# Attention, an MLP in Strassen form and a gated MLP on one core: GpSimd splits the second weight and Moe2's weights, and products take their data in pairs

## The chip, the cores and the metric

The kernel runs on one core of a Trainium2 chip. The metric is the device time of one execution in microseconds (us); the kernel before takes 808.46 us, the median of 3 runs (808.29 to 809.04). A core has a matrix engine (TensorE, PE in the rows; PEld is its weight load), a vector engine (VectorE, DVE), an activation engine (ScalarE, ACT), a general engine (GpSimd, POOL), and a queue engine (SyncE, SP) that here issues every DMA. Each engine executes its own list of instructions in order and waits for the others on semaphores.

## What is computed

```python
# stage 1: attention, B=4, H=8, S=576, D=64, causal window of 128, ALiBi bias
scores = scale * q @ k.T ; scores = where(mask, scores + bias, -1e9)
attn = exp(scores - max) ; attn = attn / (sum(attn) + 1e-9) ; out = attn @ v
x = out as (4, 576, 512)
# stage 2: Moe
h = (x.T @ U @ V).T ; u = x + h                 # rank 32
x = u + maximum(u @ w_ch1, 0) @ w_ch2           # 512 -> 2048 -> 512
# stage 3: Moe2
h = maximum(x @ w_in, 0) ; u, v = halves of h   # 512 -> 1024
v_n = (v - mean(v)) / sqrt(var(v) + 1e-6)
v_s = einsum('ts,bsd->btd', w_spatial, v_n) + b_spatial
out = (u * v_s) @ w_out
```

## The kernel before, in words

All matrix products from stage 2 on are done on fp32 numbers that are split in two: a high part (a copy into a reduced format) and a low part (the number minus its high part). A product is three matmuls: high by high, low weight by high data, high weight by low data. So each operand, data and weight, needs two passes before it can be used, a copy and a subtraction.

**The phases.** First comes attention, 16 pairs of heads, in `step`, a pipeline over three pairs. Then "up" (`u @ w_ch1`) in 24 units (G = 3 groups of 768 tokens, 8 units each), then "down" (`relu(...) @ w_ch2`) in 3 groups, then Moe2 for 4 batches. Up and down each use seven half-sized products in place of eight (Winograd's form of Strassen). The products are numbered m = 1 to 7. For them sums of blocks are needed, on the data side (`x_sum`, `r_sum`) and on the weight side: four sums S1 to S4 beside the blocks A11, A12, A22.

**Up.** A unit s is seven products of 6 matmuls, in the order (s,1), (s-1,4), (s-1,3), (s,2), (s,6), (s,5), (s,7). Between them ScalarE copies partial sums out of PSUM (`keep_p`, L934, into `sums_u`), VectorE adds and writes the four result blocks of a unit to a stage of two slots (`c11`, `c12`, `c22`), ScalarE the fourth (`c21`), and SP stores the stage to DRAM (`store_r(s)`, L421). A slot is free only when the store of two units before has landed (`room`, which waits for `r_out`): `c11(s)` waits for it, `c22(s)` stands behind `c11(s)` on VectorE, and product (s,3) waits for `c22(s)`. At the change of a group (units 8 and 16) VectorE also makes the sums and low parts of the new group's data (`x_sum`, `lo_xs`, L1271).

**The second weight.** In units 9 to 14, 17 and 18 (`W2_UNIT`) one eighth of `w_ch2` is loaded into `w1raw`. VectorE makes its four sums, ScalarE the high parts into `w2_top` (`w2_shi_of` L925, `w2_hi_of` L918, L919), VectorE the low parts, and SP stores all to DRAM (`store_w2`, `w_scr`). `w2_top` is one buffer: ScalarE waits for `w2_out` (the stores of the eighth before) at the head of `w2_shi_of`, and the `keep_p(s, 6)` of the unit stands behind it on ScalarE.

**Down.** At the end of up, the results of the first group come back from DRAM (`load_raw`, blocks a, b, d into `tok`, c into `raw_c`), the weight parts into `w2q[m]` (2 MB each), and `u` into `u_in`. For each of 8 parts kk of a product, ScalarE writes the high part (`hi_r`) and VectorE the low part (`lo_r`) of 384 columns into a ring of 5 (`rk`), and TensorE does 6 matmuls. The sums `r_sum` go by halves of 4 parts, 1536 columns; the first (`r_sum(0, 3, 0)`, L1405) stands right behind the fourth `lo_r` of the first product and reads `raw_c`. `add_res` (L1429) needs `u_in`.

**Moe2.** Its 17 weight pieces are loaded late (in the last group of down) into `w1raw`, four slots. ScalarE copies the high part (`hi_wc`, L984), GpSimd subtracts (`lo_wc`, L710). Beside this GpSimd has only the low parts in attention and, late, some of `v`. In each batch: `half_v`, `half_u`, `spatial`, `output`.

The order on each engine is that of the code below: nothing is scheduled by a planner.

Of the kernel before, what the change touches and what calls it, by code (L numbers as in the profile page):

```python
# [42 lines left out]
RING = 5  # L43
# [20 lines left out]
def rows(t):  # L64
    return P if t < TILES - 1 else TAIL
# [23 lines left out]
DN_AT = {x: (n + 1) * UNITS for n, x in enumerate(DN)}  # L89
ENTRY = {x: n * UNITS for n, x in enumerate(DN)}  # L90
ENTRIES = [(g, m, kk) for g, m in DN for kk in range(UNITS)]


W2_UNIT = {9: 0, 10: 1, 11: 2, 12: 3, 13: 4, 14: 5, 17: 6, 18: 7}
W2_AT = {kk: s for s, kk in W2_UNIT.items()}
# [3 lines left out]
def program(nc, qk, v_n, mu, mv, w1, w2, w_in, w_sp, b_sp, w_out, out_t, u_scr, r_scr, w2_scr, x2_scr):  # L99
    ctx = ExitStack()  # L100
    with ctx:
# [40 lines left out]
        pu.close()  # L142
        pl = ExitStack()
        pl.enter_context(nc.sbuf_tensor("gap1", [P, 15744], F32))
        late = sb(pl, "late", [P, 2, 4, HT], F32)
# [4 lines left out]
        w2q = {4: sb(pd, "w2q4", [P, 2, UNITS, QP], F32R)}  # L150
        raw_c = sb(pd, "raw_c", [P, UNITS, HT], F32)
        u_in = sb(pd, "u_in", [P, 2, 2, HT], F32)
        sums_d = sb(pd, "sums_d", [P, 3, 2, HT], F32)
        pd.enter_context(nc.sbuf_tensor("gap2", [P, 896], F32))
        rk = sb(pd, "rk", [P, RING, 2, HT], F32R)
        for m in (3, 1, 2, 6, 5, 7):
            w2q[m] = sb(pd, f"w2q{m}", [P, 2, UNITS, QP], F32R)
# [9 lines left out]
        wsh = sb(pc, "wsh", [P, TILES, S], F32R)  # L167
        wsl = sb(pc, "wsl", [P, TILES, S], F32R)
# [48 lines left out]
        w2q_in = {m: sem(f"w2q_in{m}") for m in range(1, 8)}  # L217
# [5 lines left out]
        w2_out = sem("w2_out")  # L223
# [11 lines left out]
        pool_passed = sem("pool_passed")  # L235
# [66 lines left out]
        vl_pad = sem("vl_pad")  # L302
# [40 lines left out]
        def r_stage(s, n=slice(0, 4)):  # L343

            if s >= LATE:
                return late[:, s % 2, n, :]
            return tok[:, n, s % 2 * HT:(s % 2 + 1) * HT]
# [10 lines left out]
        def w2_sums(kk):  # L358
# [4 lines left out]
                  tok[:, 0:4, 2 * HT:2 * HT + QP]]  # L363

# [4 lines left out]
        def _(sp):  # L369
# [31 lines left out]
            for r in range(4):  # L401
                sp.dma_start(mvraw[r * RANK:(r + 1) * RANK, :], mv).then_inc(mix_in, 16)
            load_qk(0, 2)
            load_w1(0)
            load_qk(0, 3)
            load_v(0, 2)
            load_w1(1)
# [15 lines left out]
            def load_w2(kk):  # L423
# [4 lines left out]
                else:  # L428
                    sp.wait_ge(w2_out, 6 * 16 * (kk - 1))
# [4 lines left out]
            def store_w2(kk):  # L434
                sp.wait_ge(w2_slow, kk + 1)
                sp.wait_ge(w2_low, 2 * (kk + 1))
                ra, rb = w2_of(kk)
                low = [ra[:, 0:QP], rb.rearrange("p (q c) -> p q c", c=QP), w2_sums(kk)]
                for h, parts in ((0, w2_top), (1, low)):
                    sp.dma_start(w2_scr[A11, :, h, kk, :], parts[0]).then_inc(w2_out, 16)  # L440
                    sp.dma_start(w2_scr[A12:A22 + 1, :, h, kk, :].rearrange("q p c -> p q c"),
                                 parts[1]).then_inc(w2_out, 16)
                    sp.dma_start(w2_scr[S1:S4 + 1, :, h, kk, :].rearrange("q p c -> p q c"),
                                 parts[2]).then_inc(w2_out, 16)

            def load_w2q(m):
                sp.dma_start(w2q[m][:].bitcast(F32), w2_scr[WEIGHT[m]]).then_inc(w2q_in[m], 16)
# [6 lines left out]
            def next_raw(g, n, h):  # L454

                last = {"a": (g - 1, 5), "b": (g - 1, 7), "c": (g - 1, 3), "d": (g - 1, 4)}[n]
                sp.wait_ge(rk_lo, ENTRY[last] + 4 * h + 4)
# [27 lines left out]
            def load_wc(m):  # L485
                slot = m % 4
# [1573 lines left out]
```

## Time and profile before

| | |
|---|---|
| median of 3 runs | 808.46 us |
| the profiled execution: time, span | 811.25 us, 809.5 us |
| busy PE, DVE, ACT, POOL | 91%, 61%, 47%, 12% |
| mean granted TensorE clock | 0.966 |
| moved by DMA | 119.20 MB, mean 147 GB/s |

The profile's picture of the span in 40 slices (20.2 us each; digits are tenths busy; PEclk is the granted TensorE clock in tenths of full speed):

```profile
PE   8999999889998788895589999979879999999998
DVE  6877787877675566321586896795827436416422
ACT  5977787635443343322235455536535233342322
POOL 1611136700000000000000000121331010000100
PEclk9999999999999899898779999999999999999999
DMA  6433242345368876599855625623460010000101
```

Slices 1 to 7 are attention, 8 to 18 up, 19 to 29 down, 30 to 40 Moe2. A matmul's end is modelled, so a PE that is 9 in ten may still have small holes, but where the digit is under 9, TensorE stood still.

### The profile page before, as it was taken

Reading aid. Unit: us, or ns where it says so; the run is one execution under the profiler, and the core shown is the slowest. Engines: PE = TensorE matmul, PEld = TensorE weight load, DVE = VectorE, ACT = ScalarE, POOL = GpSimd, SP = SyncE. Lnnn points to the kernel's source line nnn. Section 1 sums busy time; section 2 is a strip of 40 time slices with the busy share of each in tenths; the row PEclk is TensorE's granted clock in tenths of the full one; section 3 lists DMA queues with packets and bytes.
Section 4 is the critical chain, followed back from the end, with each engine's and each line's share of the span. In section 5 each row is a group of like instructions: output and inputs, shape, how many; then the busy total and the mean of one; then the engine's idle time right before and its main releaser. Section 6 shows DMA issues by size and latency. Waiting matters only on the chain.

```text
span 809.5 us, 13413 instructions
## 1 busy us (share of the span) xinstructions
PE 739.8 (91%) x4688; PEld 678.3 (84%) x4688; DVE 491.4 (61%) x1149; ACT 377.8 (47%) x889; POOL 97.5 (12%) x77
## 2 busy tenths in 40 slices
PE   8999999889998788895589999979879999999998
PEld 5777777789997778894589989969869899899998
DVE  6877787877675566321586896795827436416422
ACT  5977787635443343322235455536535233342322
POOL 1611136700000000000000000121331010000100
PEclk9999999999999899898779999999999999999999
DMA  6433242345368876599855625623460010000101
GB/s 205 124 110 103 88 152 73 130 156 183 120 234 279 284 241 206 192 384 421 313 183 191 195 77 197 246 65 121 131 247 1 1 60 1 25 34 0 58 0 59
DMA packets 74547, 119.20 MB, mean 147 GB/s; under 512 B 4992, under 2 KB 56704, under 8 KB 73600
## 3 DMA queue, kind: packets, MB, share of 16 engines
q1 hardware_dynamic: 74496, 118.55, 42.7%
q8 instruction: 29, 0.48, 0.2%
q14 instruction: 22, 0.18, 0.1%
HBM read 70.82 MB, written 47.71 MB: 146 GB/s over the span
## 4 chain that ended last, share of the span: by engine, by line
PE 70%; DVE 10%; DMA 10%; issue 4%; SPq 3%; ACT 3%; POOL 0%; DVEq 0%; ACTq 0%
PE bank L1840 4%; PE bank L1841 4%; PE bank L1842 4%; PE bank L1682 4%; PE wide L1697 3%; PE bank L1878 3%; PE bank L1880 3%; PE bank L1879 3%; PE bank L1989 2%; PE bank L1664 2%; DMA w_scr<-tok 2%; PE bank L1991 2%; PE bank L1990 2%; PE bank L1807 2%; PE bank L1805 2%
## 5 line engine op out<-in xcount | busy, mean ns | idle before, releaser
L1840 PE MATMUL bank<-xs,w1s 128*128 128x384 f32 x336 | 118.7, 353 | 20.0 <-ACT sums_u L934 15.8
L953 ACT ACTIVATE rk<-tok 128x384 fp32r<-128x384 f32 x144 | 73.6, 525 | 97.5 <-PE wide L1880 48.7
L1841 PE MATMUL bank<-xs,w1s 128*128 128x384 f32 x336 | 116.7, 347 | 0.0
L1842 PE MATMUL bank<-xs,w1s 128*128 128x384 f32 x336 | 116.5, 347 | 0.0
L1878 PE MATMUL bank<-rk,w2q 128*128 128x384 f32 x208 | 73.1, 351 | 32.0 <-DVE rk L1393 28.3
L1840 PEld LDWEIGHTS bank<-xs,w1s 128*128 128x128 f32 x336 | 66.4, 198 | 24.4 <-ACT sums_u L934 18.3
L796 ACT ACTIVATE sc<-sc,mn 128x256 f32<-128x256 f32 (+1 forms) x144 | 67.0, 468 | 20.7 <-DVE mn L1167 20.6
L934 ACT ACTIVATE sums_u<-bank 128x384 f32<-128x384 f32 x72 | 35.2, 489 | 83.0 <-PE bank L1842 80.0
L1878 PEld LDWEIGHTS bank<-rk,w2q 128*128 128x128 f32 x208 | 40.2, 193 | 37.5 <-DVE rk L1393 30.5
L1880 PE MATMUL bank<-rk,w2q 128*128 128x384 f32 x208 | 71.1, 342 | 0.0
L1879 PE MATMUL bank<-rk,w2q 128*128 128x384 f32 x208 | 71.1, 342 | 0.0
L1841 PEld LDWEIGHTS bank<-xs,w1s 128*128 128x128 f32 x336 | 66.6, 198 | 0.0
L1842 PEld LDWEIGHTS bank<-xs,w1s 128*128 128x128 f32 x336 | 66.4, 198 | 0.0
L1396 DVE TENSOR_TENSOR rk<-tok,rk 128x384 fp32r<-128x384 f32 x96 | 51.0, 564 | 23.0 <-ACT rk L953 23.0
L710 POOL TENSOR_TENSOR wvl<-w1raw,wvh 128x512 fp32r<-128x512 f32 x4 | 7.5, 1896 | 362.8 <-ACT wvh L984 362.8
L1167 DVE CUSTOM_DVE_ANT_0 sc<-bank,bias 128x256 f32<-128x256 f32 (+1 forms) x128 | 42.3, 384 | 5.4 <-PE bank L1644 3.5
L1176 DVE COPY pt<-bank 128x512 f32<-128x512 f32 x48 | 31.4, 682 | 20.8 <-PE bank L1682 20.8
L1878 PE MATMUL wide<-rk,w2q 128*128 128x384 f32 x128 | 43.3, 338 | 0.6 <-DVE rk L1396 0.5
L1880 PE MATMUL wide<-rk,w2q 128*128 128x384 f32 x128 | 43.0, 336 | 0.0
L1879 PE MATMUL wide<-rk,w2q 128*128 128x384 f32 x128 | 43.0, 336 | 0.0
L1879 PEld LDWEIGHTS bank<-rk,w2q 128*128 128x128 f32 x208 | 40.3, 194 | 0.0
L1880 PEld LDWEIGHTS bank<-rk,w2q 128*128 128x128 f32 x208 | 40.2, 193 | 0.0
(222 smaller groups left out, 1830.7 us busy)
## 6 DMA issues: line engine op xcount, KB each, us to landing
r_scr<-tok SPq DMA_DIRECT2D x19, 768.0 KB, 4.1
w2q<-w_scr SPq DMA_DIRECT2D x7, 2048.0 KB, 14.5
tok<-r_scr SPq DMA_DIRECT2D x18, 768.0 KB, 5.8
qkraw<-qk SPq DMA_DIRECT2D x32, 288.0 KB, 3.0
w1raw<-w SPq DMA_DIRECT2D x32, 256.0 KB, 3.7
w_scr<-tok SPq DMA_DIRECT2D x12, 512.0 KB, 3.5
u_scr<-tok SPq DMA_DIRECT2D x6, 768.0 KB, 4.6
raw_c<-r_scr SPq DMA_DIRECT2D x6, 768.0 KB, 4.6
```

What stands on the lines that cost most here:

```text
L796: act.activation(w, w, ACT.Exp, bias=mn[:, s, n:n + 1], scale=-1.0, accum_out=sm[:, i, c:c + 1]).then_inc(exp_done, 1)
L934: act.activation(sums_u[:, i, :], a_ps[s % 2][:, 0:HT], ACT.Copy).then_inc(kept, 1)
L953: act.activation(rk[:, n % RING, 0], raw[RAW_OF[m]][:, kk, :], ACT.Relu if m <= 3 else ACT.Copy).then_inc(rk_hi, 1)
L1167: dve.tensor_tensor_reduce(out=out, in0=src, in1=add, scale=-SCALE, scalar=3e38, op0=ALU.add, op1=ALU.min, accum_out=mn[:, s, n:n + 1]).th ...
L1396: dve.tensor_tensor(lo, x, hi, ALU.subtract).then_inc(rk_lo, 1)
L1682: last = pe.transpose(pt_ps[f % 2][:, j * P:(j + 1) * P], sc[:, i % 2, n, w * P:(w + 1) * P], ident[:, :])
L1840: pe.matmul(o, wh, ah, start=(k == 0 and m in FRESH), stop=False, skip_group_check=True)
L1841: pe.matmul(o, wl, ah, start=False, stop=False, skip_group_check=True)
L1842: last = pe.matmul(o, wh, al, start=False, stop=(k == 1), skip_group_check=True)
L1878: pe.matmul(o, wh, rh, start=(kk == 0 and m in FRESH), stop=False, skip_group_check=True)
L1879: pe.matmul(o, wl, rh, start=False, stop=False, skip_group_check=True)
L1880: last = pe.matmul(o, wh, rl, start=False, stop=(kk == UNITS - 1), skip_group_check=True)
```

## The change

- The second weight is no longer split on ScalarE and VectorE but wholly on GpSimd, in `split_w2`: 4 sums, 4 copies, 4 subtractions. It runs through the eighths by itself, as soon as its semaphores allow, from the end of unit 8's sums on. `W2_UNIT` now says only where SP stores an eighth. `store_w2` stores in two parts (blocks, then sums), and the load of the eighth after next stands behind the store.
- Moe2's 17 weight pieces are loaded and split during attention: GpSimd does copy and subtraction (`split_wc`) between its other work there, SP stores both parts to a new DRAM buffer `wc_scr`, and in the last group of down they come back ready, both parts together (`load_group`). That is twice the bytes of before at this place. `hi_wc` and `lo_wc` are gone.
- Down takes its data in pairs: `hi_r` and `lo_r` work on 768 columns, for two parts kk, in a ring of 3 pairs. The sums `r_sum` go by 768 columns and are spread by two tables, `FIRST_T` (first group) and `NEXT_T`; the first of them now stands behind the seventh pair.
- The join of up and down: the order of loads on SP, and the places in memory; ScalarE makes the high parts of the first three pairs before the last `keep_p` of up.
- At the join of attention and up: three low parts (`xs`, m = 7, 5, 4) go from GpSimd to VectorE, and three of the four last `mix_up` move from unit 2 to units 2, 3 and 4.

```diff
-RING = 5
+RING = 3
+DP = UNITS // 2
+SLOTS = 9
-W2_UNIT = {9: 0, 10: 1, 11: 2, 12: 3, 13: 4, 14: 5, 17: 6, 18: 7}
+W2_UNIT = {9: 0, 10: 1, 11: 2, 12: 3, 13: 4, 15: 5, 16: 6, 18: 7}
+WC_AFTER = {0: [0, 1], 1: [2, 3], 2: [4], 3: [5, 6], 4: [7, 8, 9], 5: [10, 11, 12], 6: [13], 7: [14, 15, 16]}
+FIRST_T = {(2, 2): [(3, 0)], (2, 3): [(3, 1), (2, 0)], (6, 0): [(2, 1), (4, 0)], (6, 1): [(3, 2), (2, 2)],
+           (6, 2): [(3, 3), (2, 3)], (6, 3): [(1, 0), (4, 1)], (5, 0): [(1, 1), (4, 2)],
+           (5, 1): [(1, 2), (4, 3)], (5, 2): [(1, 3)]}
...
             def store_w2(kk):
-                sp.wait_ge(w2_slow, kk + 1)
                 sp.wait_ge(w2_low, 2 * (kk + 1))
...
+                sp.wait_ge(w2_slow, 2 * (kk + 1))
+                for h, four in ((0, w2_top[2]), (1, w2_sums(kk))):
+                    sp.dma_start(w2_scr[S1:S4 + 1, :, h, kk, :].rearrange("q p c -> p q c"),
+                                 four).then_inc(w2_out_s[kk % 2], 16)
...
                 if s in W2_UNIT:
                     kk = W2_UNIT[s]
-                    if kk >= 1 and kk + 1 < UNITS:
-                        load_w2(kk + 1)
                     store_w2(kk)
+                    if kk + 2 < UNITS:
+                        load_w2(kk + 2)
...
+            def split_wc(m):
+                slot, w = m % SLOTS, DM if m < WS else S
+                x, hi = wprep[:, slot, 1, 0:w], wprep[:, slot, 0, 0:w].bitcast(F32R)
+                pool.wait_ge(weights_in[slot], 16 * (m // SLOTS + 1 + (m == n_wc - 1)))
+                pool.tensor_copy(hi, x).then_inc(wc_hi, 1)
                 pool.wait_ge(wc_hi, m + 1)
+                if m < n_wc - 1:
+                    pool.tensor_tensor(x.bitcast(F32R), x, hi, ALU.subtract).then_inc(wc_ready, 1)
...
+            def split_w2(kk):
...
+                pool.tensor_tensor(s[:, 0], ra[:, QP:2 * QP], rb[:, QP:2 * QP], ALU.add).then_inc(w2_sum, 1)
+                pool.tensor_tensor(s[:, 2], ra[:, 0:QP], ra[:, QP:2 * QP], ALU.subtract).then_inc(w2_sum, 1)
...
+                if kk:
+                    pool.wait_ge(w2_out_t, 4 * 16 * kk)
+                pool.tensor_copy(w2_top[0].bitcast(F32R), ra[:, 0:QP]).then_inc(w2_hi, 1)
+                pool.tensor_copy(w2_top[1].bitcast(F32R), pair).then_inc(w2_hi, 1)
...
+            for kk in range(UNITS):
+                split_w2(kk)
...
-                if s in W2_UNIT:
-                    w2_shi_of(W2_UNIT[s])
-                    w2_hi_of(W2_UNIT[s])
...
+                if s == NU - 1:
+                    for n in range(RING):
+                        hi_r(n)
                 keep_p(s, 7)
...
-                if m == 1 and g == 0 and kk % 4 == 3:
-                    r_sum(0, 3, kk // 4)
...
+                for t, k in FIRST_T.get((m, j), []) if g == 0 and m != 4 else []:
+                    r_sum(0, t, k)
+                ahead = g + 1 if m == 4 else g
+                for t, k in NEXT_T.get((m, j), []) if 0 < ahead < G else []:
+                    r_sum(ahead, t, k)
```

What this does to the order of instructions is shown at three places. The first is ScalarE in unit 10 of up; `sums_u` is the copy that TensorE waits for (`keep_p`), `tok<-tok`, `tok<-wst` and `tok<-w1raw` are high parts of the second weight. Before:

```order
L941 ACTIVATE tok<-bank 128x384
L925 ACTIVATE tok<-wst 128x4x256
L918 ACTIVATE tok<-w1raw 128x256
L919 ACTIVATE tok<-w1raw 128x2x256
L934 ACTIVATE sums_u<-bank 128x384 x3
```

ScalarE now, from unit 14 over the change of group at units 15 and 16 (`xs` is the high part of the new group's data):

```order
L1005 ACTIVATE sums_u<-bank 128x384 x3
L1012 ACTIVATE tok<-bank 128x384
L954 ACTIVATE xs<-tok 128x768 x2
L1005 ACTIVATE sums_u<-bank 128x384
L954 ACTIVATE xs<-tok 128x768
```

The three weight copies between the block result and the partial sums are gone; nothing of the second weight is left on this engine.

The second place is GpSimd behind attention, where its list ended before. This is one eighth of the second weight, and it comes 8 times:

```order
L776 TENSOR_TENSOR tok<-w1raw 128x256
L777 TENSOR_TENSOR tok<-w1raw 128x256
L779 TENSOR_TENSOR tok<-tok,w1raw 128x256
L781 TENSOR_TENSOR tok<-w1raw,tok 128x256
L784 CAST tok<-w1raw 128x256
L785 CAST tok<-w1raw 128x2x256
L787 TENSOR_TENSOR w1raw<-w1raw,tok 128x256
L790 TENSOR_TENSOR w1raw<-w1raw,tok 128x512
L796 CAST tok<-tok 128x2x256 x2
L801 TENSOR_TENSOR tok<-tok 128x2x256 x2
```

Twelve instructions (two lines stand for two each) stand here where there was nothing, all on one engine. Two of the casts and two of the subtractions are on the sums, the others on the blocks.

The third place is VectorE at the join of up and down. `late` is the result stage of the last units, `rk<-tok,rk` is `lo_r`, `tok<-raw_c,tok` the first `r_sum`. Before:

```order
L1386 TENSOR_TENSOR late<-bank,sums_u 128x384
L1393 SCALAR_TENSOR_TENSOR rk<-tok,rk 128x384 x4
L1405 SCALAR_TENSOR_TENSOR tok<-raw_c,tok 128x1536
L1393 SCALAR_TENSOR_TENSOR rk<-tok,rk 128x384
L1374 TENSOR_TENSOR late<-bank,sums_u 128x384
```

Now:

```order
L1393 TENSOR_TENSOR late<-bank,sums_u 128x384
L1400 SCALAR_TENSOR_TENSOR rk<-tok,rk 128x768 x3
L1381 TENSOR_TENSOR late<-bank,sums_u 128x384
L1387 TENSOR_SCALAR late<-late 128x384
L1400 SCALAR_TENSOR_TENSOR rk<-tok,rk 128x768 x4
L1412 SCALAR_TENSOR_TENSOR tok<-raw_c,tok 128x768
L1433 TENSOR_TENSOR sums_d<-sums_d,u_in 128x384 x2
```

The sum that reads `raw_c` has moved from behind 4 parts (half a product) to behind 7 pairs (14 parts), and the last unit's result now comes ahead of it.

## Rows read from the trace of the kernel before

**Rows 1.** Windows, whole core: stretch, its length, busy time per engine, PE clock, DMA share, GB/s

```profile
230.80:331.90 101.10, 83.53 (x422) 80.68 (x421) 56.72 (x105) 39.43 (x71) 0.00 (x0) 0.90 0.73 247
331.90:370.00 38.10, 34.77 (x199) 34.16 (x199) 10.58 (x22) 10.49 (x23) 0.00 (x0) 1.00 0.88 330
370.00:413.00 43.00, 23.75 (x108) 22.75 (x109) 20.62 (x29) 9.72 (x20) 0.00 (x0) 0.72 0.88 353
413.00:586.90 173.90, 162.30 (x913) 157.47 (x913) 134.38 (x210) 90.39 (x181) 18.66 (x12) 1.00 0.46 148
586.90:619.00 32.10, 27.74 (x154) 24.37 (x152) 12.83 (x29) 12.98 (x25) 10.98 (x8) 0.95 0.44 156
```

**Rows 2.** Timeline of PE in up: start, length, instruction; 15 matmuls, first and last

```profile
160.69 0.34 PE L1840 MATMUL bank<-xs,w1s 128*128 128x384 f32 x1
...
163.12 0.34 PE L1842 MATMUL bank<-xs,w1s 128*128 128x384 f32 x1
```

**Rows 3.** Who PE waited for, 0 to 600 us: total, times, longest

```profile
PE bank L1878 <- DVE rk L1393: 28.3, 11, 12.9
PE bank L1840 <- ACT sums_u L934: 15.8, 7, 3.9
PE wide L1805 <- ACT vr L1081: 4.2, 1, 4.2
...
PE wide L1751 <- DVE tok L1216: 2.4, 1, 2.4
```

**Rows 4.** Chain that ended last, units 10 and 11: start, length, piece

```profile
243.54 0.40 ACT tok L918
...
254.20 0.40 ACT tok L918
```

**Rows 5.** Chain at the join of up and down

```profile
374.44 12.57 DMA raw_c<-r_scr
...
392.16 13.16 DMA u_in<-u_scr
```

**Rows 6.** Chain at the entry of Moe2

```profile
583.10 6.53 DMA w1raw<-w_sp
```

**Rows 7.** Groups by line on POOL: count, busy, mean ns of one

```profile
L694 POOL TENSOR_TENSOR wst<-wst,w1raw 128x256 f32<-128x256 f32 x1 | 0.7, 734 | 0.0
...
L698 POOL TENSOR_TENSOR w1s<-w1raw,w1s 128x512 fp32r<-128x512 f32 x1 | 1.3, 1282 | 0.0
...
L714 POOL IOTA dist<- 128x256 f32 x1 | 0.3, 347 | 0.0
```

**Rows 8.** Timeline of DVE: one sum beside busy POOL, one beside idle POOL

```profile
150.79 2.06 DVE L1301 TENSOR_TENSOR wst<-w1raw 128x256 f32<-128x256 f32 x1
...
158.87 0.41 DVE L1301 TENSOR_TENSOR wst<-w1raw 128x256 f32<-128x256 f32 x1
```

**Rows 9.** Timeline of PE: start of product (7,3), two products into unit 8

```profile
222.98 0.44 PE L1840 MATMUL bank<-xs,w1s 128*128 128x384 f32 x1 [0.52 <-DVE tok L1386]
```

**Rows 10.** DMA issues on the page: count, KB each, median us to landing

```profile
r_scr<-tok SPq DMA_DIRECT2D x19, 768.0 KB, 4.1
```

**Rows 11.** Groups by line on DVE: 768 columns, 1536 columns

```profile
L1271 DVE TENSOR_TENSOR xs<-tok,xs 128x768 fp32r<-128x768 f32 x14 | 13.2, 952 | 4.2 <-ACT xs L869 4.2
...
L1415 DVE SCALAR_TENSOR_TENSOR tok<-tok 128x1536 f32<-128x1536 f32 x6 | 10.5, 1753 | 0.3
```

**Rows 12.** Chain in attention: the same piece of three steps in a row

```profile
15.77 1.66 PE wide L1697 x16
...
23.58 1.66 PE wide L1697 x16
...
31.39 1.66 PE wide L1697 x16
```

**Rows 13.** Timeline of POOL in attention: first and last of the six between

```profile
24.81 0.73 POOL L691 TENSOR_TENSOR wst<-w1raw 128x256 f32<-128x256 f32 x1
...
28.92 0.74 POOL L701 TENSOR_TENSOR w1s<-w1raw,w1s 128x256 fp32r<-128x256 f32 x1
```

More of the change, by code:

```diff
@@ L363, in program, with wc_total, wc_loads @@
                   tok[:, 0:4, 2 * HT:2 * HT + QP]]
+        def wc_total(slot):
+            return 16 * len(range(slot, n_wc, SLOTS))
+        def wc_loads(slot):
+            return wc_total(slot) + 16 * (slot == (n_wc - 1) % SLOTS)
         block = ctx.enter_context(nc.Block())
@@ L585, in _ @@
                 load_u(g, 22)
-                if g == G - 1:
-                    for m in range(4):
-                        load_wc(m)
                 next_raw(g, "d", 0)
@@ L593, in _ @@
                 load_u(g, 12)
+                if g == G - 1:
+                    for slot in range(SLOTS):
+                        sp.wait_ge(wc_out[slot], wc_total(slot))
+                    sp.wait_ge(rk_used, DN_AT[(g, 1)])
+                    load_group(range(0, WU))
                 store_x2(g, 11)
-                if g == G - 1:
-                    for m in range(WU, WO):
-                        load_wc(m)
-                else:
+                if g < G - 1:
                     next_raw(g + 1, "a", 0)
@@ L744, in _ @@
             pool.tensor_tensor(mvl[:, :], mvraw[:, :], mvh[:, :], ALU.subtract).then_inc(mix_ready, 1)
+            for m in WC_AFTER[0]:
+                split_wc(m)
             lo_x(0, 0)
             first_w1()
-            lo_x(0, 1)
-            with pool.Fori(1, B - 1) as b:
-                for i in range(PAIRS):
-                    lo_x(*((b, i - 2) if i >= 2 else (b - 1, i + 2)))
+            for p in range(1, (B - 2) * PAIRS + 2):
+                lo_x(*divmod(p, PAIRS))
+                for m in WC_AFTER.get(p, []):
+                    split_wc(m)
             lo_x(B - 2, 2)
@@ L999, in _ @@
             step(B - 1, 0)
+            for slot in range(SLOTS):
+                act.wait_ge(wc_out[slot], wc_total(slot))
             hi_xs(0, 1)
@@ L1053, in _ @@
                     hi_xs(g + 1, 7)
-            for n in range(len(ENTRIES)):
-                g, m, kk = ENTRIES[n]
-                if n >= RING and ENTRIES[n - RING][2] == UNITS - 1:
+            for n in range(RING, len(ENTRIES)):
+                g, m, j = ENTRIES[n]
+                if ENTRIES[n - RING][2] == DP - 1:
                     ended = ENTRIES[n - RING][0:2]
@@ L1928, in _ @@
             up(NU - 1, 3)
-            down(0, 1, range(2, UNITS))
+            down(0, 1, range(2, DP))
             for g, m in DN[1:]:
```

464 lines of the change are left out of this document (212 added, 252 removed).

## The prediction

> **What bounds the kernel now.** The windows by stage come first, since TensorE is busy over 90% of the span and only the stages in which it isn't can give time. What it should need is counted in matmuls: from the first to the last of 15 are 2.43 us, 0.1736 us each at full clock [rows 2]. Up and down have the same 1008 matmuls each, 42 to a unit of up (7.29 us), 6 to a part of down (1.04 us). Against that the windows show [rows 1]:
>
> - 230.8 to 331.9, ten units with the second weight beside them: 101.1 us for 72.9, an excess of 28.2, at clock 0.90;
> - 331.9 to 370, the last 33 products of up: 38.1 for 34.4, excess 3.7;
> - 370 to 413, 18 sixes of matmuls at the join: 43.0 for 18.7, excess 24.3, at clock 0.72;
> - 413 to 586.9, 152 sixes: 173.9 for 158.3, excess 15.6;
> - 586.9 to 619, the entry of Moe2: 32.1 at clock 0.95.
>
> Next, who TensorE waited for [rows 3]: ScalarE's partial sums 15.8 us, VectorE's `rk` 28.3 (one wait of 12.9), `vr` at the entry of Moe2 4.2, and a `mix_up` 2.4. Last, the chain of waits says why. With the second weight the same ScalarE copy comes round every 10.66 us, 243.54 and 254.20 [rows 4], where a unit is 7.29: stores of `w2_top` land, ScalarE copies, VectorE subtracts, SP stores, and TensorE's `keep_p` stands in ScalarE's list behind the wait. At the join two DMAs stand in the chain, `raw_c` 12.57 us and `u_in` 13.16 us [rows 5], each with VectorE's low parts queued behind. At the entry of Moe2 it is `w_sp` [rows 6], for which ScalarE waits ahead of `vr`.
>
> **The second weight.** ScalarE and VectorE lose all of it, so the loop of rows 4 is cut. Its successor is GpSimd. A sum or subtraction of 256 columns is 0.734 us there, of 512 is 1.282 [rows 7]. Copies on GpSimd are not in this trace. An eighth is 5 operations of 256, 3 of 512 (3.67 + 3.85 = 7.5 us), and copies of 256, 512, 512 and 512. From below the nearest row is `iota`, 0.347 for 256, at most twice that for 512: 0.35 + 3 x 0.69 = 2.4. From above it is the subtraction, 0.73 + 3 x 1.28 = 4.6. So an eighth is 9.9 or 12.1 us; I take 9.9, a copy reading one operand like nothing else here but being simpler than the two-operand form. Both are longer than a unit, 7.29, so what counts is the head start.
>
> GpSimd starts when the sums of unit 8 are done, some 226.4 us. Product (7,3) starts at 222.98 [rows 9], two products into unit 8, whose end was 7.8 later, less two products: unit 9 begins at 228.7 and unit s at 228.7 + 7.29 (s - 9). Eighth kk is ready at 226.4 + 9.9 (kk + 1). SP waits for it, and `store_r(s)` stands behind it: with two stores and two loads issued first (2.4) and the store's landing (4.1, [rows 10], and 1.5 for what is queued ahead), the slot is free 8 us after the eighth. It must be free when `c22(s+2)` is wanted, 1 us into unit s+3. For kk = 0 to 4 (units 9 to 13) the slot is free at 244.3, 254.2, 264.1, 274.0, 283.9 and wanted at 251.6, 258.9, 266.2, 273.4, 280.7: late by 0.6 and then, beyond it, 2.6. That is 3.2 us. Units 14 and 17 have no eighth, and GpSimd catches up there.
>
> The second cost is VectorE's. One sum with both operands in SBUF took 2.06 us beside a busy GpSimd and 0.41 beside an idle one [rows 8]: it waited for a whole GpSimd instruction. The Trainium skill, "SBUF — State Buffer", Who interferes with whom, says the same of the shared port pair, that the second to issue blocks until the first is through; the trace agrees in its 1.65 us. At the change of group at units 15 and 16, eight such VectorE instructions stand in a row in the chain, and GpSimd is now busy all through. Each waits one GpSimd instruction, 9.9 / 12 = 0.8 us: 6.5 us. The old excess of 1.2 there stays, as does 1.0 for the slow clock after a wait. Sum: 3.2 + 6.5 + 1.2 + 1.0 = 11.9 us of excess where there were 28.2, a gain of 16.3. By the upper price the slots of kk = 2, 3 and 4 are late by 4.5, 4.8 and 4.8 (14.1), eighths 5 and 6 add some 5, VectorE's row 8 x 1.0, and with 1.2 and 1.0 the excess is 29: a gain of nothing. I book 15. The Trainium skill, "GPSIMD Engine Reference", Elementwise — side-by-side cycle accounting, gives 1.03 cycles an element for bodies of few operations; at 1.2 GHz that is an estimate of 0.44 us for 512 columns ahead of the fixed part, and the eighth would be about 9.5 us.
>
> **The join of up and down.** Now `raw_c` is first read behind 7 pairs, that is 7 x 2.08 = 14.6 us of TensorE's time after the start, and its load is issued some 4 us after it; even at the old 12.6 us [rows 5] it is about on time, and less is queued ahead. `u_in` is issued behind the store of the last unit and before 4 MB of weights: issued at +12, behind 2 MB, landed at +16.5, wanted at +15. That leaves a stall of 1.6. The start itself waits 2.4 (partial sum, block, low part of a pair). What is late next is VectorE: `r_sum` and low part of 768 columns are 0.9 us each (952 ns, 1753 ns for twice the columns [rows 11]), and in the first group seven pairs have two sums: 2.7 us against TensorE's 2.08, plus 1 us for `add_res` and `dc` each. Written out pair by pair with a ring of 3 that is 7.5 us of stalls. Sum for the first group: 1.6 + 2.4 + 7.5 = 11.5. The later two groups have the same sums over more pairs; I keep the 2.5 each that the change of group costs now. The end of down keeps 1.5, its weight copies on ScalarE and GpSimd being gone. All: 18 of excess, where 24.3 + 15.6 and 2 us of the window before were 41.9. Gain 24; I book 23. Bounds: nothing at all beside the start's 2.4 gives 35 at most, the old chain at half its cost 12.
>
> **The smaller parts.** The last units of up waited for stores queued behind six loads; four are there now: 1.5. The `mix_up` wait of 2.4 goes, since its block is asked for a unit later; the three low parts on VectorE are about as long as what they waited for GpSimd before: 2.5 booked. At the entry of Moe2 the wait of 4.2 and the slow clock (5% of 32.1, 1.6) go: 5.5 booked. The 9 MB of ready parts that now come back are spread from the first product of the last group on, and `ws` (3 MB) has 26 us. Attention gets 17 times about 2 us of GpSimd work and 14 MB of DMA. The rows bear on it: the same piece of three steps stands at 15.77, 23.58 and 31.39, that is 7.81 us apart each time [rows 12], and in the second step GpSimd ran six instructions without a pause [rows 13]. So GpSimd work beside attention is hidden by TensorE; I book a loss of 1 (bounds 0.5 and 6, the latter 12 steps times half of a 1 us wait).
>
> **Sum.** 15 + 23 + 1.5 + 2.5 + 5.5 - 1 = 46.5. The profiled execution took 811.25 (span 809.5), so 764.75; the median of the runs lies 2.8 below it: 762.
>
> **Rivals.**
>
> 1. GpSimd's eighth is 12 us (copies as dear as subtractions). For it: every line of work on GpSimd with an operand read costs 2.3 ns a column and more. Against: `iota`. The gain of 15 goes: 777. Chance 0.13.
> 2. The join stays the bound: VectorE's sums, or the DMA queue (330 and 353 GB/s over the two windows, 28 MB), hold TensorE as before in half of the excess. For it: DMA share 0.88 in both windows [rows 1]. Gain 12 in place of 23: 773. Chance 0.13.
> 3. VectorE is held up by GpSimd in attention also. For it the rows of 2.06 and 0.41 [rows 8]; in each of 12 steps three short instructions (`sums`) could wait for one each, up to 2.5 us, less the 1.2 us that VectorE idles: 16 us, 778. Against it rows 12 and 13. The rule of the Trainium skill named above speaks for it. Chance 0.05.
> 4. It gets slower. One mechanism: the second weight on a single engine. SP's store of results stands behind the eighth, so TensorE runs at GpSimd's pace. Seven eighths end at 226.4 + 7P, and the slot behind the seventh is wanted at 302.5: the stall is 7P - 59 with the 8 us of storing and 9 of VectorE's instructions. It eats the 28.2 and the other 31.5 when P = 17 us. Copies would have to cost 9.5 us an eighth, or 5.3 ns a column, twice a subtraction's. At P = 18.5, 819 us. Chance 0.06.
>
> The forecast has the rest, 0.63. Its own range is 752 to 772, and the cases 1 to 3 reach to 778, so that I say 748 to 789 with some room for two at once. Within 0.2% (1.6 us, about what a measurement of this kernel can tell from no change) needs several rivals together: 0.03. Slower 0.07, faster 0.90.
>
> **What the new profile would show.** `sums_u` gone from TensorE's waits in units 9 to 18, and the stretch from the start of (8,3) ten units on near 84 us, not 101. GpSimd's casts of 512 columns at 0.6 to 0.7 us and an eighth in about 10. `raw_c` and `u_in` gone from the chain, the first 18 sixes of down in under 28 us at clock 1.0, and waits for `rk` of 0.5 to 2 us each, spread over products 2, 6 and 5 of the first group. `half_v` without a wait for `vr`. Attention's steps as far apart as now. Wrong I would be if casts are over 1.2 us, if TensorE's largest waits in units 11 to 16 are for blocks whose slot is not free, or if the steps of attention with splits beside them are longer.

## The result, and the profile after

| | before | after |
|---|---|---|
| median of runs | 808.75 us (4 runs, 808.29 to 810.34) | 775.17 us (4 runs, 773.02 to 775.82) |
| ratio | | 0.9577, 95% interval 0.9554 to 0.9600 |
| profiled execution, span | 811.25, 809.5 us | 773.02, 771.2 us |
| mean granted TensorE clock | 0.966 | 0.982 |

The kernel became faster by 33.6 us. The forecast was 762.0 us (748 to 789): the direction and the range were right, the value 13 us too low.

The stages of after come first, cut at the same marks as [rows 1] and with the stretch ahead of them: the start of up, product (8,3), ten units further, the first product of down, its third product, `half_v`, `spatial`. The columns are those of [rows 1].

```profile
150.35:230.54 80.19, 74.84 (x416) 72.05 (x415) 59.73 (x110) 37.60 (x69) 4.60 (x4) 0.98 0.50 171
230.54:315.63 85.09, 76.95 (x422) 75.88 (x421) 36.83 (x51) 24.73 (x47) 81.19 (x94) 0.94 0.85 287
315.63:354.45 38.82, 34.48 (x200) 34.19 (x199) 11.08 (x22) 11.44 (x22) 0.00 (x0) 0.99 0.92 344
354.45:384.87 30.42, 23.53 (x108) 22.84 (x109) 11.76 (x16) 6.22 (x9) 0.00 (x0) 0.79 0.88 355
384.87:554.85 169.98, 161.61 (x914) 157.84 (x913) 128.52 (x163) 71.97 (x96) 0.00 (x0) 1.00 0.56 185
554.85:580.78 25.93, 25.72 (x153) 23.19 (x153) 12.92 (x29) 9.91 (x20) 3.48 (x2) 1.00 0.80 307
```

Against [rows 1]: the ten units 101.1 to 85.1, the last 33 products 38.1 to 38.8, the first 18 sixes of down 43.0 to 30.4, the rest of down 173.9 to 170.0, the entry of Moe2 32.1 to 25.9. In the ten units VectorE fell from 56.7 to 36.8 us busy and GpSimd rose from 0 to 81.2, almost the whole stretch. The first 18 sixes are the only stretch left with a clock under 0.9, at 0.79. (A six is the 6 matmuls of one part.)

Who TensorE waited for, 0 to 600 us of after (total, times, longest):

```profile
PE bank L1876 <- DVE rk L1400: 11.2, 2, 6.9
PE bank L1837 <- DVE tok L1393: 8.7, 4, 5.3
PE bank L1876 <- DVE rk L1403: 6.2, 9, 1.4
PE wide L1748 <- DVE tok L1255: 2.4, 1, 2.4
...
PE bank L1837 <- ACT sums_u L1005: 1.0, 2, 0.8
```

Against [rows 3]: ScalarE's partial sums fell from 15.8 to 1.0, `rk` from 28.3 to 17.4, and `vr` is gone. The block `c22` (L1393), whose slot of the stage must be free, grew from 1.0 (L1386 in before) to 8.7. New is a load of attention's data (`qkraw`), 0.9. The `mix_up` wait of 2.4 is still there.

**The second weight now.** GpSimd's timeline shows one eighth, from its first sum to the first sum of the next (start, length, instruction):

```profile
267.50 0.73 POOL L776 TENSOR_TENSOR tok<-w1raw 128x256 f32<-128x256 f32 x1
...
270.86 0.61 POOL L785 CAST tok<-w1raw 128x512 fp32r<-128x512 f32 x1
...
272.13 1.28 POOL L790 TENSOR_TENSOR w1raw<-w1raw,tok 128x512 fp32r<-128x512 f32 x1
273.37 1.16 POOL L796 CAST tok<-tok 128x512 fp32r<-128x512 f32 x2
274.50 2.50 POOL L801 TENSOR_TENSOR tok<-tok 128x512 fp32r<-128x512 f32 x2
276.96 0.72 POOL L776 TENSOR_TENSOR wst<-w1raw 128x256 f32<-128x256 f32 x1
```

It is 9.46 us for 9.9 forecast; a copy of 512 columns takes 0.61. The two eighths at the change of group take 12.2 and 14.4 (from 276.96 and from 289.19). SP's timeline gives the pace at which results are stored in those units:

```profile
241.66 0.54 SPq L480 DMA_DIRECT2D r_scr<-tok  x1
251.03 0.54 SPq L480 DMA_DIRECT2D r_scr<-tok  x1
...
270.99 0.55 SPq L480 DMA_DIRECT2D r_scr<-tok  x1
280.89 1.24 SPq L480 DMA_DIRECT2D r_scr<-tok  x2
```

With the one left out (261.55) they are 9.4 to 10.5 us apart, where a unit is 7.3: SP keeps GpSimd's pace. The chain of waits says how that reaches TensorE (start, length, piece):

```profile
275.53 3.75 DMA w_scr<-w1raw
279.29 0.34 SPq L491
279.68 1.06 SPq L491
280.89 5.03 DMA r_scr<-tok
286.05 0.56 DVE tok L1375
286.60 1.52 DVE xs L1310
...
291.44 0.48 DVE tok L1393
291.96 0.69 PE bank L1837
```

An eighth's stores must land before SP may load the next but one into their place (L491). The store of the unit's results stands behind both and takes another 5.03. Only then does VectorE go on, after it stood idle for 3.88: with a block (L1375) and three instructions of the change of group (L1310, L1327, L1310), behind which stands the block that TensorE needs (L1393). These three take 4.86 us here. At the 0.95 that each takes alone (experiment 6) they would take 2.9, so 2.0 of the wait of 5.31 are VectorE's and the rest is its late start.

**The join now.** The same view at the start of down:

```profile
339.69 12.60 DMA r_scr<-late
...
353.44 0.88 DVE rk L1400
354.45 0.66 PE bank L1876
...
364.82 8.14 DMA r_scr<-late
373.04 6.11 DMA u_in<-u_scr
```

`raw_c`, the 12.57 of [rows 5], is gone, and `u_in` fell from 13.16 to 6.11. Ahead of each of TensorE's two waits (4.34 at 354.45, 6.89 at 381.12) there is a store of results which takes 12.60 and 8.14 us to land. Before has three rows to set beside this: its chain at the same place, its list of DMA issues (count, KB, median us to landing), and TensorE's wait behind `u_in`:

```profile
355.97 12.28 DMA r_scr<-late
```

```profile
r_scr<-late SPq DMA_DIRECT2D x5, 768.0 KB, 10.0
```

```profile
406.89 0.69 PE L1878 MATMUL bank<-rk,w2q 128*128 128x384 f32 x1 [6.36 <-DVE rk L1393]
```

So the slow store is not new, only its share in a wait (before started down with waits of 1.54 and 1.79), and the wait behind `u_in` is as long as before. One thing is new: `u_in` now lies where the last stage of up lies, so SP waits for the last store to land before it loads `u_in`. In before that wait stood behind this load, which was issued 2 us behind the store (390.21 and 392.16).

In attention the chain of after has the same piece of three steps at 58.67, 67.21 and 75.75, 8.54 us apart each. In before they stand at 58.00, 66.54 and 75.08, 8.54 apart as well, so the split of Moe2's weights beside them costs TensorE nothing there. The 0.67 us by which after is late were there at 39.87 already (39.20 in before): at 35.05 TensorE waited 0.90 for `qkraw`, a load that SP issued behind the store of a split piece and the load of the next.

### The profile page after: what moved, and what is told of

It reads as the page before. It is cut to its first block, busy times and chain, and to the rows that moved or that the text cites. A ratio compares the mean times of both kernels' runs of the same rounds, so it can differ in the third digit from the quotient of the medians.

```text
span 771.2 us, 13217 instructions
## 1 busy us (share of the span) xinstructions
PE 728.5 (94%) x4688; PEld 671.2 (87%) x4688; DVE 454.9 (59%) x1036; ACT 339.0 (44%) x764; POOL 180.3 (23%) x187
## 4 chain that ended last, share of the span: by engine, by line
PE 68%; DVE 12%; DMA 7%; POOL 5%; issue 4%; ACT 3%; SPq 1%; DVEq 0%; ACTq 0%; POOLq 0%
PE bank L1837 4%; PE bank L1839 4%; PE bank L1838 4%; PE bank L1679 3%; PE wide L1694 3%; PE bank L1876 3%; DMA r_scr<-late 3%; PE bank L1877 3%; PE bank L1878 3%; PE bank L1985 2%; PE bank L1987 2%; PE bank L1986 2%; PE bank L1804 2%; PE bank L1802 2%; PE bank L1803 2%
## 5 line engine op out<-in xcount | busy, mean ns | idle before, releaser
L1837 PE MATMUL bank<-xs,w1s 128*128 128x384 f32 x336 | 115.9, 345 | 9.9 <-DVE tok L1393 8.7
L1839 PE MATMUL bank<-xs,w1s 128*128 128x384 f32 x336 | 114.6, 341 | 0.0
L1838 PE MATMUL bank<-xs,w1s 128*128 128x384 f32 x336 | 114.6, 341 | 0.0
L868 POOL TENSOR_TENSOR vl<-vr,vh 128x512 fp32r<-128x512 f32 x8 | 11.3, 1407 | 401.5 <-ACT vh L1146 401.5
L1022 ACT ACTIVATE rk<-tok 128x768 fp32r<-128x768 f32 x72 | 60.6, 847 | 91.5 <-PE wide L1878 30.4
L1876 PE MATMUL bank<-rk,w2q 128*128 128x384 f32 x208 | 72.1, 347 | 18.4 <-DVE rk L1400 11.2
L1005 ACT ACTIVATE sums_u<-bank 128x384 f32<-128x384 f32 x72 | 35.4, 491 | 101.1 <-PE bank L1839 95.9
L1837 PEld LDWEIGHTS bank<-xs,w1s 128*128 128x128 f32 x336 | 65.0, 193 | 12.5 <-DVE tok L1393 9.9
L1877 PE MATMUL bank<-rk,w2q 128*128 128x384 f32 x208 | 70.5, 339 | 0.0
L1878 PE MATMUL bank<-rk,w2q 128*128 128x384 f32 x208 | 70.5, 339 | 0.0
L1838 PEld LDWEIGHTS bank<-xs,w1s 128*128 128x128 f32 x336 | 65.0, 193 | 0.0
L1839 PEld LDWEIGHTS bank<-xs,w1s 128*128 128x128 f32 x336 | 64.8, 193 | 0.0
L1403 DVE TENSOR_TENSOR rk<-tok,rk 128x768 fp32r<-128x768 f32 x48 | 45.4, 953 | 24.5 <-ACT rk L1022 24.0
```

What stands on the lines that cost most here:

```text
L1005: act.activation(sums_u[:, i, :], a_ps[s % 2][:, 0:HT], ACT.Copy).then_inc(kept, 1)
L1022: act.activation(rk[:, n % RING, 0], raw[RAW_OF[m]][:, 2 * j:2 * j + 2, :], ACT.Relu if m <= 3 else ACT.Copy).then_inc(rk_hi, 1)
L1403: dve.tensor_tensor(lo, x, hi, ALU.subtract).then_inc(rk_lo, 1)
L1837: pe.matmul(o, wh, ah, start=(k == 0 and m in FRESH), stop=False, skip_group_check=True)
L1838: pe.matmul(o, wl, ah, start=False, stop=False, skip_group_check=True)
L1839: last = pe.matmul(o, wh, al, start=False, stop=(k == 1), skip_group_check=True)
```

## The experiments

"Stage" means the length of a stretch between the marks above in the profiled execution; ratios are to the kernel before, from runs on the same chip. After itself was not run again beside the experiments. Before took 808.75 us beside after and 810.4 to 810.8 beside them, so a difference from after in us is good to about 2 us, and the stages say more. The ten units, where an edit does not touch them, took 84.7 to 85.8.

### 1. GpSimd's eighth made short

```diff
-  pool.tensor_copy(w2_top[1].bitcast(F32R), pair)
+  pool.tensor_copy(w2_top[1][:, :, 0:8].bitcast(F32R), pair[:, :, 0:8])
...
```

(the other copies and all subtractions but the 256-column one in the same way)

> The changed kernel with GpSimd's share of the second weight made short: 6 of its 12 instructions an eighth, the copies and subtractions of A12/A22 and of the sums and the copy of A11, work on 8 columns in place of 256 or 512 (this part of the second weight is then not split). Waits, stores and loads stay. An eighth goes from about 10 us to about 5. Theory (GpSimd's pace and its grip on VectorE's reads cost the 12.2 us of excess in the ten units from (8,3) on): the three waits for a block's slot or for the sums (0.98, 1.86, 5.31 us) and the slow clock behind the last go, the ten units take 75 to 78 us in place of 85.1, the whole is 7 to 9 us faster, 767. Rival (the DMA queue, 0.95 to 0.99 busy there, holds the store of results, and GpSimd does not matter): the waits stay, under 2 us.

Measured: 768.10 us (766.70 to 771.26), ratio 0.9498 (0.9450 to 0.9545). The ten units took 80.49, and waits of 0.68 and 3.84 for the block stay. Both theories miss: GpSimd was busy 39.7 us of the stretch and no longer 81, and still SP stored results 8.0 to 9.9 us apart.

GpSimd's timeline has the reason, waits in each eighth but the first for stores that free the one `w2_top`:

```profile
257.59 0.19 POOL L784 CAST tok<-w1raw 128x8 fp32r<-128x8 f32 x1 [0.91 <-DMA w_scr<-w1raw]
```

So taking half of GpSimd's busy time away is worth 4.6 us of this stretch. VectorE's instructions of 768 columns took 0.95 to 1.26 there, so what is left is hardly its slowing; by these rows it goes by landings of stores and SP's order.

### 2. `u_in` loaded early

```diff
-  u_in = sb(pd, "u_in", [P, 2, 2, HT], F32)
+  u_in = w1raw[...]            # room that is free here
...
+  sp.wait_ge(u_out[0], 16 * G); sp.wait_ge(u_out[1], 16 * G)
+  load_u(0, 11); load_u(0, 12)
   sp.wait_ge(up_p, UP_AT[(NU - 1, 3)])
```

(the same two loads removed behind the last store)

> u_in in w1raw (free by then) in place of the memory of the last stage, and the first two loads of u issued ahead of raw_c and of the last unit's store. Theory (of the 30.4 us of the join, 6.9 is a wait for u_in, whose load stands behind the landing of the last store): the 6.89 us wait at 381 goes, VectorE reaches the sums up to 7 us earlier, and part of it comes back as waits for VectorE's sums of 0.5 to 1.5 us; the whole 4 to 7 us faster, 769 to 771. Rival 1 (VectorE's sums are the limit from the start of product 2 on, so that an earlier u_in only moves the wait): under 2 us. Rival 2 (raw_c comes later by the 0.8 MB ahead of it and takes the place): 0 to 3 us.

Measured: 764.64 us (762.94 to 766.68), ratio 0.9450 (0.9402 to 0.9498). The stage went from 30.42 to 21.20 and its clock from 0.79 to 0.93; the wait of 6.89 is gone. It gives 10.5 us by the medians, 9.2 of them in this stage: more than the wait, since the slow matmuls behind it go too. This one load is the largest single part of the miss.

### 3. Fewer loads ahead of the late stores

```diff
-  for m, ago in ((1, 21), (2, 22), (6, 23)):
+  for m, ago in ((1, 21), (2, 23)):
-  if s == LATE + 2: load_raw(0, "d", 0) ...
+  if s == LATE + 3: load_raw(0, "d", 0) ...
+  load_w2q(6)                  # behind the last store
   load_w2q(5)
```

> Order of loads at the end of up: block d in unit 22, w2q2 in unit 23, w2q6 only behind the last store, so that the store of unit 21 stands behind 2 MB in place of 3.7. Theory (the 4.34 us wait at the start of down is this store, 12.6 us to landing, for whose slot VectorE waits 5.5 us): the wait shrinks to about 2.4 (partial sum, block, first low part) with the clock drop behind it, the whole 2 to 5 us faster. Rival (the queue is full either way and something else lands last): within 1 us, or slower by 1 to 3 where w2q2 or d is late.

Measured: 773.91 us (772.88 to 775.59), ratio 0.9564 (0.9519 to 0.9608), less than 0.2% from after. The wait at the start of down shrank from 4.34 to 2.68, and VectorE got its slot 9.7 us after the store was issued, for 12.6: what is queued ahead of a store does lengthen it. But the two waits for `rk` grew together from 11.2 to 14.3, the second to 11.60. The 2 MB that were moved now stand ahead of `u_in`. While `u_in` is late, nothing ahead of it pays.

### 4. The last `mix_up` one product later

```diff
-  elif (s, m) == (4, 2):
+  elif (s, m) == (4, 3):
       mix_up(B - 1, 3, bank[6:8])
```

(its addition on VectorE moves from unit 4 to 5)

> The last mix_up moves from behind (4,2) to behind (4,3) in unit 5, its addition on VectorE to unit 5. Theory (the 2.36 us wait of unit 4 and the low clock after it, 4.8 us of excess in that unit, come from the third addition standing behind c11(4), which waits for the product just ahead of the mix_up): the wait goes or is under 0.5, unit 4 loses 4 to 5 us, the whole 3 to 5 us faster. Rival (the wait reappears at the new place or ScalarE's first copy of the last weight unit, which waits for it, is late): within 1 us.

Measured: 771.41 us (767.52 to 772.97), ratio 0.9532 (0.9488 to 0.9577). The stretch from the start of up to (8,3) went from 80.19 to 76.22, the wait of 2.36 is gone. In other kernels with this code unchanged the stretch was 78.7 (three times) and 80.2 (four times), by the clock behind the wait, so the edit gives 2.4 to 4.

### 5. VectorE's sums in the first group made short

```diff
-  a, b, c, d = (raw[n][:, u, :] for n in "abcd")
+  a, b, c, d = (raw[n][:, u, 0:HT if g else 8] for n in "abcd")
```

> It leaves out part of the computation: in the first group of down (g = 0), VectorE's sums of two results of up take 8 columns of 384, so that each costs little over its fixed part. Everything else, the transfers too, is as in the changed kernel. Theory A (the prediction's term): the sums hold TensorE in the first group. The seven waits for rk there, 0.38, 1.42, 1.43, 0.53, 0.38, 0.44 and 0.44 us, 5.0 in all, go; the stretch from the start of down to product (0,6) falls from 30.42 to about 25.5 and the time by 4 to 5 us, to some 770.5. Rival B: the waits are paid to the low parts and the block's own operations of VectorE, or to the load of u_in; the stretch stays above 29 and the time falls by less than 1.5 us.

Measured: 767.72 us (764.27 to 769.14), ratio 0.9471 (0.9424 to 0.9518). All seven waits for L1403 in the first group are gone, but not where I looked, since they lie behind the mark at 384.87 (387.58 to 406.37): the 18 sixes took 30.23, and the rest of down went from 169.98 to

```profile
383.19:546.08 162.89, 159.50 (x914) 157.93 (x913) 117.99 (x161) 71.33 (x95) 0.00 (x0) 1.00 0.58 193
```

that is, 7.1 us less. The third and the fourth product of down took 8.3 us each in place of 13.2 and 10.5. Theory A holds in mechanism, with the right place one stage later and 7.1 in place of 5.

### 6. GpSimd silent at the change of group

```diff
-  W2_UNIT = {9: 0, 10: 1, 11: 2, 12: 3, 13: 4, 15: 5, 16: 6, 18: 7}
+  W2_UNIT = {9: 0, 10: 1, 11: 2, 12: 3, 13: 4, 17: 5, 18: 6, 19: 7}
+  if kk == 5:
+      pool.wait_ge(xs_lo, 7 * G)
   split_w2(kk)
```

> GpSimd pauses between eighth 4 and eighth 5 of the second weight until VectorE has made the seven low parts of the change of group, and the three last eighths are stored in units 17, 18 and 19 in place of 15, 16 and 18. Theory A (contention): the waits for tok of 1.86 and 5.31 us at the change of group come from VectorE's operations, which take 1.1 to 1.8 us beside a busy GpSimd and 0.95 alone, and from GpSimd's eighth, stretched from 10 to 14 us. With GpSimd silent both shrink: ten units in 85.1 - 5 = 80 us, time about 770. Rival B (queue of the stores): the wait of 5.31 is for a slot freed by the store behind eighths 3 and 4, which this doesn't move; the ten units stay above 83.5, and the three late eighths meet the loads of the join, so that the time is the same within 1.5 us.

Measured: 773.48 us (771.02 to 775.22), ratio 0.9543 (0.9494 to 0.9593). The ten units shrank to 81.32 and the next stretch grew from 38.82 to 44.19, with waits of 2.60 and 6.83, since the last eighth ended at 321.9. In time that is rival B, nearly nothing, while the ten units are nearer to A's 80 than to B's 83.5. That they shrank is no proof of contention, since the edit also took the eighths' stores out of units 15 and 16, ahead of the stores of results (experiment 9 separates the two). But it shows VectorE's instructions at this place alone (first fence) and beside GpSimd in after (second):

```profile
285.10 0.96 DVE L1329 TENSOR_TENSOR tok<-tok 128x768 f32<-128x768 f32 x1
285.98 0.95 DVE L1312 TENSOR_TENSOR xs<-tok,xs 128x768 fp32r<-128x768 f32 x1
```

```profile
288.24 1.80 DVE L1327 TENSOR_TENSOR tok<-tok 128x768 f32<-128x768 f32 x1
289.97 1.47 DVE L1310 TENSOR_TENSOR xs<-tok,xs 128x768 fp32r<-128x768 f32 x1
```

The eight of them in after's 276 to 294 us sum to 11.1 us; at 0.95 each they would be 7.6.

### 7 and 8. The edits together

Number 7 has the edits of 2, 3 and 4; number 8 those of 2 and 4.

> Three edits at once: u_in in room of its own, loaded ahead of raw_c; raw_d a unit later and the loads of two weight parts moved; the last mix_up a product later. Theory A (each removes its own wait): 775.2 - 10.5 - 3.8 = 760.9, and with the wait for u_in gone the moved loads are worth what they took from the wait at the start of down, 4.34 - 2.68 = 1.7, since the later wait can't grow in their place: 759.2. Rival B: the waits pass the time on to the next one; what the moved loads give, the first group of down takes back, and the time is 761 or more, not under that of the same kernel without the moved loads.

> As the kernel with three edits, without the moved loads: only the earlier u_in and the later mix_up. Theory A (two separate waits): 775.2 - 10.5 - 3.8 = 760.9, between 759 and 763; up start to (8,3) 76.2, down start to (0,6) 21.2, both as in the single runs. Rival B (they share a resource): units finished earlier leave GpSimd's eighths and SP's stores as late as now, so that the 4 us won in unit 4 come back as longer waits for tok at units 12 to 16; the ten units take 88 to 89 in place of 85.1 and the time is 764.5.

Measured: 759.15 us (756.23 to 761.58), ratio 0.9348 (0.9298 to 0.9397), and 762.91 us (761.32 to 764.36), ratio 0.9412 (0.9364 to 0.9460). (Number 7's profiled execution, the slowest of its four, took 79.26 in the first stretch, with a wait of 2.32 for the first unit's partial sum that no other run with the edit shows; why is open.) Number 8 lies 12.3 below after for the 14.3 of the single edits added; the first stretch is that of the single run (76.19), the ten units stayed at 84.71, so rival B of number 8 (88 to 89) is out, and of the 2 us that lack 1.1 is in the 18 sixes (22.32 for 21.20). The moved loads, flat alone, give 1.9 in their own stage (39.08 to 37.16) once `u_in` no longer stands behind them; the intervals of the two kernels overlap, so I take this from the stage and not from the medians.

### 9. The store of results ahead of the eighth's

```diff
-  W2_UNIT = {9: 0, 10: 1, 11: 2, 12: 3, 13: 4, 15: 5, 16: 6, 18: 7}
+  W2_UNIT = {9: 0, 10: 1, 12: 2, 13: 3, 15: 4, 16: 5, 18: 6, 19: 7}
```

> The changed kernel with one table altered: eighths 2 to 7 of the second weight are stored in units 12, 13, 15, 16, 18 and 19 in place of 11, 12, 13, 15, 16 and 18. So SP stores a unit's results before it waits for the eighth that ends later, and GpSimd works as before. Theory A (the prediction's slot term): the waits for tok of 1.0, 1.9 and 5.3 us in units 13 to 16 are for slots of results whose store stands behind an eighth's stores and loads; they shrink to what VectorE takes beside GpSimd, so that the ten units take 79 to 81 us in place of 85.1, and the time falls by 3 to 5 us, to some 771, if nothing is late further on. Rival B (VectorE beside GpSimd): with the store in time, VectorE's low parts of the change of group, 1.1 to 1.8 us each, still end as late; ten units 84 to 85, time 775.

Measured: 768.68 us (767.55 to 770.85), ratio 0.9482 (0.9458 to 0.9506). The two stretches are (the second was 38.82 in after):

```profile
229.91:308.44 78.53, 75.25 (x421) 74.12 (x421) 36.79 (x51) 24.96 (x47) 74.58 (x86) 0.98 0.84 285
308.44:349.88 41.44, 34.79 (x200) 34.18 (x199) 10.99 (x22) 11.32 (x22) 6.50 (x8) 0.96 1.01 370
```

Waits for the block fell from 8.7 to 2.6 (two others, 0.76 and 0.45, are new). GpSimd works as much as in after, and VectorE beside it is stretched nearly as much: the same eight instructions of 768 columns take 10.6 us, for 11.1 in after. Yet the stretch is shorter than in experiment 1, where GpSimd works half as long. So most of the excess was the place of the store of results in SP's list. Of the 6.6 us, 2.6 come back at the start of down, where the wait grew from 4.34 to 6.27.

### 10. All of it

The edits of 7 and 9.

> The kernel with three edits and the altered table together. Theory A: its 759.2 less 4 to 5 us in units 13 to 16, 755, with waits of under 2 us at the change of group. Rival B: the two last eighths, stored in units 18 and 19, push the first loads of results and weights for down back, and the wait at the start of down grows from 2.7 by as much; ten units shorter but the next stretch longer, the time 759 within 1.5.

Measured: 754.37 us (5 runs, 752.63 to 755.37), ratio 0.9299 (0.9275 to 0.9323). It beats both kernels: 7.0% below before, 20.8 us below after. Stages:

```profile
150.26:226.44 76.18, 73.08 (x416) 70.47 (x415) 59.44 (x110) 37.58 (x69) 4.62 (x4) 1.00 0.52 180
226.44:305.41 78.97, 75.16 (x421) 74.23 (x421) 38.57 (x51) 24.94 (x47) 74.58 (x86) 0.98 0.84 284
305.41:343.13 37.72, 34.77 (x199) 34.16 (x199) 11.08 (x22) 11.32 (x22) 6.53 (x8) 1.00 1.00 366
343.13:365.99 22.86, 20.59 (x108) 20.12 (x108) 13.15 (x17) 6.88 (x10) 0.00 (x0) 0.93 0.93 368
```

Here the next stretch is 37.7, 0.6 over number 7's, so theory A holds. The time is not all won: at the third product of down TensorE now waits 2.27 for its weight part (`w2q<-w_scr`), one of the loads that were moved behind the last store (1.46 in number 7).

## Why the prediction was right, and where its sum was off

The terms, each against the stages of the two profiled executions (us; up starts at 149.68 in before and 150.35 in after):

| term | booked | measured |
|---|---|---|
| second weight, ten units | 15 | 16.0 |
| join and down | 23 | 16.5 |
| last units of up | 1.5 | -0.7 |
| `mix_up` and the junction | 2.5 | 0.9 |
| entry of Moe2 | 5.5 | 6.2 |
| attention | -1 | -0.7 |
| sum | 46.5 | 38.2 |
| from the profiled execution to the median | -2.75 | +2.15 |

The 13.2 us of the miss are 8.3 of the terms and 4.9 of the last line: before's profiled execution lay 2.5 to 2.8 above its median, after's 2.15 below. I take that as chance between single executions, which scatter by more (before's own ranged from 806.05 to 815.46 beside the experiments).

**Second weight: right in price and size, its parts shared out wrongly.** The iota's bound was the right one (an eighth 9.46 for 9.9, a copy of 512 at 0.61, [rows 7]), and the excess was 12.2 for 11.9. That the totals agree is in part luck. The waits for the block cost 8.15 (0.98, 1.86, 5.31) where I had 3.2 for slots, and VectorE's eight instructions beside GpSimd stretched by 3.5 where I had 6.5; 2.0 of the 3.5 lie inside the wait of 5.31, so the two do not add up. The first was too small because I let GpSimd catch up in unit 14; its eighths at the change of group stretched instead, from 9.5 to 12 and 14 us. The second was too large because an instruction of VectorE did not wait for a whole one of GpSimd: 1.0 to 1.8 us for 0.95 and not the 2.06 for 0.41 of [rows 8], which stood beside a GpSimd instruction of 1.9 us. Experiment 9 shows the slot term: with the store ahead, the waits fall to 2.6. By the prediction's own last sentence this was a sign of being wrong: TensorE's largest waits in units 11 to 16 are for blocks whose slot is not free. The term was in the sum, but at 3.2 for some 6 (8.15 less the 2.0).

**Join and down: the step that failed is "that leaves a stall of 1.6" for `u_in`.** I had it issued 12 us after the start of down, landed at 16.5 and wanted at 15. The last unit's store was issued at 10.4 and took 8.14 us to land, where I had both done by 12, so `u_in` was issued at 18.6 (373.04) and took 6.11: landed at 24.7, wanted at 19.8. Two readings failed there. I had used the landing of [rows 10], a median over calmer stretches, for a store with weights and blocks queued ahead of it, when before's list of DMA issues has 10.0 for the stores of just this stage. And I counted `u_in` as issued behind the store, where the changed kernel waits for it to land; before's own wait there, 6.36, had told what a late `u_in` costs. Experiment 2 prices the step at 10.5 us with the slow clock behind it. The sign I gave for this place, the first 18 sixes in under 28 us at clock 1.0, came out at 30.4 and 0.79. The other term of this stage was good: VectorE's sums at 7.5 forecast, 7.1 in experiment 5. The start (whose wait the table counts with the last units of up) waited 4.34 for 2.4, behind a landing of 12.60. In experiment 3, with fewer loads ahead, it waited 2.68, and the time stayed the same, since `u_in` was later still.

**Last units of up.** "Four are there now" counted loads; what mattered was the landing of the one store that the start of down waits for, 12.60 for 12.28. This stretch ends with that wait of 4.34, where before had 1.54 and 1.79. Booked +1.5, it is -0.7.

**`mix_up`.** "The wait goes" failed: TensorE waited 2.36 at 192.72 for 2.40 at 177.39 in before. The wait moved with the `mix_up` and kept its length, because in both kernels the addition it needs stands on VectorE behind the same list: two blocks of the unit and three low parts of the first weight (L1348, L1357, L1360; L1309, L1318, L1321 in before). One product later (experiment 4) it costs nothing. The 0.9 won in this stretch (81.12 to 80.19) is less than its scatter: with after's code unchanged it took 78.7 or 80.2.

**Entry of Moe2 and attention.** Both as forecast: no wait for `vr`, clock 1.00, and attention's steps apart as before. Its loss is the one wait for `qkraw`: in the chain this load stands behind the store of a piece that GpSimd had split (24.37 to 25.65), so here too GpSimd's pace reached TensorE through SP's list.

**The rivals.** 1 (eighth of 12 us) is out by 9.46. 2 (join stays the bound in half) is half true: of the excess of 41.9 there, 16.5 went in place of 23, and the cause is the queue that it names, for `u_in`'s store and load. 3 (VectorE held in attention) is out by the unchanged steps; the sharing is real only where VectorE's two-operand work fills the chain. 4 (slower) is out: GpSimd's pace does set SP's, but at 9.5 us, not 17.

## What to carry to other kernels

A queue that serves several tasks in order hands the slowest one's pace to all: what stands behind a wait in the list of transfers matters more than the arithmetic that the wait is for. Moving the store of results ahead of it (one table, no other work changed) took 6.6 us off the ten units, more than half of GpSimd's work taken away did (4.6); 2.6 of them came back at the start of down, and the two kernels' times are alike (768.68 and 768.10). For a transfer on the critical path, take its time to landing from the stretch in which it will be issued, with what is queued ahead, and not the median of the page; look which landing a load itself waits for, above all where the change gives it memory that another transfer still reads; and order edits by the wait that ends last, since a fix ahead of a later wait measures as nothing until that one is gone.

## What the runs showed of the hardware

Behind a long wait TensorE runs slow for a while. This is after's timeline behind the wait of 5.31 us:

```profile
292.45 0.52 PE L1838 MATMUL bank<-xs,w1s 128*128 128x384 f32 x1
292.77 0.52 PE L1839 MATMUL bank<-xs,w1s 128*128 128x384 f32 x1
...
295.80 0.33 PE L1837 MATMUL bank<-xs,w1s 128*128 128x384 f32 x1
295.98 0.33 PE L1838 MATMUL bank<-xs,w1s 128*128 128x384 f32 x1
```

Matmuls start 0.32 us apart until 295.5, and 0.17 apart from there, the higher of the two levels. The slow stretch was 3.6 us here and 6.1 behind the wait of 4.34 at the start of down (354.45 to 360.55). So a wait of 4 to 5 us cost 1.7 to 2.8 more. I had booked 1.0. Behind a shorter wait it went either way: the 2.36 for the `mix_up` comes in the same code in after and in experiment 1, and the granted clock of the 7.28 us behind it was 0.77 in after and 1.00 there.

VectorE and GpSimd slow each other down where both work on data in SBUF: VectorE's 768 columns took 1.0 to 1.8 us for 0.95, and GpSimd's sums of 256 columns 1.33 to 1.45 us (four in a row from 289.19) for 0.73. The Trainium skill, "SBUF — State Buffer", Who interferes with whom, says that the second to issue waits until the first is through. The traces show that both lose, VectorE up to 0.85 us an instruction here; whether the two take turns, as that rule would have it, or share within an instruction, no run here shows. Copies on GpSimd cost half of a two-operand form of the same width here (0.61 and 1.28 us for 512 columns). For the copy this agrees with the 1.03 cycles an element (an estimate of 0.44 us ahead of the fixed part) of the Trainium skill, "GPSIMD Engine Reference", Elementwise — side-by-side cycle accounting. For `tensor_tensor` the same section has about 2.6 cycles an element, an estimate of 1.11 us, and the 1.28 agrees with that.
